# Two orders changed where a group of eight pairs begins in the last stage of a fused long convolution and rational feed-forward kernel

## What is computed

```python
    h_filt = h_mlp * window
    u = x * v
    ...
    y = np.fft.irfft(Uf * Hf[None, :, :], n=L, axis=1)[:, :S, :]
    return (x * y).astype(np.float32)
...
    h = x @ w_in                       # (24960, 128) @ (128, 2048)
    h2 = h * h
    h3 = h2 * h
    P = a[0] + a[1] * h + a[2] * h2 + a[3] * h3
    Q = 1.0 + np.abs(b[0]) * np.abs(h) + np.abs(b[1]) * h2
    g = P / (Q + 1e-06)
    return (g @ w_out).astype(np.float32)
```

## Time and profile before

| | |
|---|---|
| Median of three runs | 2089.32 us (2088.35 to 2089.32) |
| Profiled execution, its own time | 2086.96 us |
| Profiled execution, span from first to last instruction | 2084.5 us |
| Mean granted TensorE clock | 0.988 |
| PE busy | 1983.6 us (95%) |
| GpSimd busy | 1872.7 us (90%) |
| VectorE busy | 1826.2 us (88%) |
| ScalarE busy | 1825.9 us (88%) |

### The profile page before, as it was taken

One profiled execution on the slowest core, in us unless ns is written; L12 is line 12 of the kernel. 1 busy time (PEld: TensorE's weight loads), 2 busy tenths in 40 slices (PEclk: granted clock), 3 DMA queues, 4 the chain that ended last, 5 costly groups with the idle time before them and its releaser, 6 DMA issues. The chain is left out here.

```text
span 2084.5 us, 33029 instructions
## 1 busy us (share of the span) xinstructions
PE 1983.6 (95%) x8964; PEld 1466.1 (70%) x8964; DVE 1826.2 (88%) x2511; ACT 1825.9 (88%) x2671; POOL 1872.7 (90%) x1218
## 2 busy tenths in 40 slices
PE   7999799999969999999999999999999999999997
PEld 5777699999946666666666666666666666666664
DVE  5888688888859999999999989999899999999997
ACT  5888566666659999999999999999999999999998
POOL 4777588888839999999999999999999999999997
PEclk9999899999979999999999999999999999999999
DMA  7999876676540111111111111111111111111100
GB/s 202 307 309 310 229 176 174 176 182 169 140 108 21 44 33 32 32 32 33 32 32 32 37 33 33 33 32 48 35 43 32 32 33 32 32 32 32 33 13 13
DMA packets 66556, 176.34 MB, mean 85 GB/s; under 512 B 5191, under 2 KB 8975, under 8 KB 63519
## 3 DMA queue, kind: packets, MB, share of 16 engines
q1 hardware_dynamic: 66407, 174.67, 30.7%
HBM read 102.89 MB, written 71.76 MB: 84 GB/s over the span
## 5 line engine op out<-in xcount | busy, mean ns | idle before, releaser
L657 POOL TENSOR_TENSOR den<-slope,mag 128x832 f32<-128x832 f32 x480 | 947.0, 1973 | 0.0
L910 PE MATMUL acc_p<-g_s,w_out_k 128*128 128x416 f32 x1920 | 768.1, 522 | 48.8 <-DVE oT L830 22.9
L789 DVE SCALAR_TENSOR_TENSOR num<-square,level,h_p 128x832 f32<-128x832 f32 x480 | 517.6, 1078 | 82.3 <-ACT square L695 43.3
L649 POOL TENSOR_SCALAR slope<-mag,den_c 128x832 f32<-128x832 f32 x480 | 499.1, 1040 | 72.3 <-DVE mag L784 49.4
L910 PEld LDWEIGHTS acc_p<-g_s,w_out_k 128*128 128x128 f32 x1920 | 340.5, 189 | 296.0 <-issue 183.2
L822 DVE SCALAR_TENSOR_TENSOR g_s<-num,ratio,r_p 128x832 f32<-128x832 f32 x480 | 517.4, 1078 | 20.0 <-ACT r_p L711 4.6
L695 ACT ACTIVATE square<-h_p,centre 128x832 f32<-128x832 f32 x480 | 469.7, 979 | 41.7 <-DVE mag L784 24.2
L899 PE MATMUL h_p<-xy_hi,w_lo 128*128 128x416 f32 x960 | 460.5, 480 | 5.5 <-DVE num L789 2.8
L704 ACT ACTIVATE den<-den 128x832 f32<-128x832 f32 x480 | 442.4, 922 | 4.6 <-issue 2.9
L711 ACT ACTIVATE r_p<-den 128x832 f32<-128x832 f32 x480 | 428.2, 892 | 0.9 <-DVE g_s L822 0.7
L899 PE MATMUL h_p<-xy_lo,w_hi 128*128 128x416 f32 x960 | 338.5, 353 | 0.0
(11 more groups left out here) (79 smaller groups left out, 2792.8 us busy)
## 6 DMA issues: line engine op xcount, KB each, us to landing
bent<-bent_s SPq DMA_DIRECT2D x60, 576.0 KB, 5.8
bin_s<-bent SPq DMA_DIRECT2D x23, 1440.0 KB, 9.7
x_s<-in_x SPq DMA_DIRECT2D x59, 416.0 KB
vin_s<-back SPq DMA_DIRECT2D x29, 768.0 KB, 6.0
back<-back_s SPq DMA_DIRECT2D x23, 960.0 KB, 7.8
v_s<-in_v SPq DMA_DIRECT2D x30, 416.0 KB
out<-o_s SPq DMA_DIRECT2D x60, 208.0 KB
pos_s<-in_pos_emb SPq DMA_DIRECT2D x30, 88.0 KB
```

Of the source, the lines that this page charges most:

```text
L649: nc.gpsimd.tensor_scalar(slope[:, q % DEEP], mag[:, q % DEEP], den_c[:, 1:2], den_c[:, 0:1], ALU.mult, ALU.add).then_inc(slope_done, 1)
L657: nc.gpsimd.tensor_tensor(den[:, q % DEEP], slope[:, q % DEEP], mag[:, q % DEEP], ALU.mult).then_inc(den_done, 1)
L789: nc.vector.scalar_tensor_tensor(out=num[:, q % NUMS], in0=square[:, q % SQUARES], scalar=level[:], in1=h_p[:, q % 2, :, 0:TOK], op0=ALU.a ...
L910: mm = nc.tensor.matmul(acc_p[:, 0:TOK], w_out_k[:, ft], g_s[:, q % DEEP, t], start=(ft == 0), stop=(ft == FT - 1))
```

## The change

At an opening (m = 0 and m = 8) two orders are changed. VectorE does `times_x` (at m = 8) and `numerator` ahead of the copy of the sums. TensorE does `turn_in` (at m = 8) and `hidden` ahead of `project`. Nothing is added or removed, and each wait stays with its instruction.

```diff
@@ VectorE, step @@
                     activation(i, q)
+                    if more and m in TIMES_X:
+                        times_x(nxt + TIMES_X.index(m), i * (BLOCKS // SLOTS) + (q // BLOCK_PAIRS + 1) // SLOTS, s, TIMES_X.index(m))
+                    if ahead:
+                        numerator(i + (q + LEAD_E) // PER, (q + LEAD_E) % PER)
                     if m in SUMS:
                         c = blk * BATCH + SUMS.index(m) - 1
                         if positive(c + 1):
                             sums(c)
-                    if more and m in TIMES_X:
-                        times_x(nxt + TIMES_X.index(m), i * (BLOCKS // SLOTS) + (q // BLOCK_PAIRS + 1) // SLOTS, s, TIMES_X.index(m))
-                    if ahead:
-                        numerator(i + (q + LEAD_E) // PER, (q + LEAD_E) % PER)
@@ TensorE, step @@
-                    project(i, q)
+                    opens = m % PAIRS == 0
+                    if not opens:
+                        project(i, q)
                     nxt, s = (blk + 1) * 2, (q // BLOCK_PAIRS + 1) % SLOTS
                     if more and m in TURN_IN:
                         turn_in(nxt + TURN_IN.index(m))
                     if ahead:
                         hidden(i + (q + LEAD_H) // PER, (q + LEAD_H) % PER)
+                    if opens:
+                        project(i, q)
```

## The result

The changed kernel took 2092.63 us in the median of 13 runs (2090.57 to 2095.75), the kernel before 2088.49 us beside it (2086.29 to 2089.74). The ratio is 1.0024, with a 95% interval of 1.0016 to 1.0032. So the change made the kernel slower by a quarter of a per cent, where 0.42% faster was forecast.

The account below looks back on a forecast made before the run. A loop of ScalarE's chain and VectorE's steps through the magnitude was taken to set block time. A 13.7 us gain at m = 8 less 4.9 at m = 0 gave 8.8 us saved, 2080.5 us, range 2074 to 2088.5.

Parts of the forecast that it names:

- m = 8, VectorE: Openings at m = 8: the copy's wait for TensorE goes, a gain of 13.7 us over 29 openings.
- m = 0, VectorE: Openings at m = 0: the magnitude comes 0.13 us late in the loop, 0.23 outside, a loss of 4.9 us.
- m = 0, TensorE: Openings at m = 0: steps end 0.63 us later, about nothing lost; from above 0.2 us each, 5.8 us.
- The sum: Whole kernel: 13.7 - 4.9 = 8.8 us saved, 2080.5 us in the median, 0.42% less.
- The half clock at every m = 0: Rival: TensorE's clock drops at m = 0 openings, costing 41 us, about 2121 us; chance 0.05.
- nothing: Rival: the copy's wait comes back as another, of ScalarE or the numerator at m = 8; 2089.3 us; chance 0.08.
- GpSimd is the bound: Rival: both GpSimd pauses at m = 8 go, saving 29.6 us, 2059.7 us; chance 0.04.
- The transposes come too late for ScalarE at m = 2: Rival: at 0.2 us each the gain falls to 3.0 us, 2086.3; at 0.3 or more none; chance 0.2.
- The clock: TensorE's idle grows to about 1.26 us at m = 0, 3.2 at loop turns; one drop costs about 1.4 us.

Follow-up runs that it names:

- changed_less_products: The changed kernel with h of pairs 7 and 8 of each block summed from two products instead of three; 2080.39 us, ratio 0.9966 to the kernel before.
- m0_only: Both new orders, VectorE's and TensorE's, at m = 0 alone, with m = 8 as in the kernel before; 2108.34 us, ratio 1.0091.

## Why the prediction was wrong

**m = 8, VectorE: right.** The copy's wait cost 0.37 us in the block that I read, and the distance from `activation` to magnitude fell by that. The run with m = 8 alone gained 14.1 us (2088.72 - 2074.58), against a term of 13.7; in its trace it is 12.8 from the stage's first `activation` to its last.

**m = 0, VectorE: right.** The magnitude came 0.14 us later, against 0.13 in the loop. Over the 26 blocks between the first, the last and the two turns of the loop, the distances from one `activation` to the next give 4.9 us, as the term did for 29.

**m = 0, TensorE: this is the step that failed.** The text had it "about nothing, but close". Its own numbers were right: TensorE idle for 0.63 us more, the transposes 0.63 us later, ScalarE's copy to `o_s` not held up. The mistake was to follow the lateness to the next engine that waits, find a margin, and stop. I took it that TensorE would catch up, from the remark that it "runs up to two pairs ahead", for which I showed no row. It does not. Of the 0.63 us it still carries 0.43 in relation to VectorE at m = 4, and in its own distances it caught up 0.06 us in four pairs: 1310.55 - 1304.31 = 6.24 us for its first instruction of the opening, 6.18 at m = 3 and 4. It has the transposes of the output at m = 0 and the products of `rows` at m = 2 on top of its pairs. At m = 4 its result is wanted with next to no margin: in the kernel before, the transposes ended at 1318.14 + 0.52 = 1318.66 and the split started at 1318.75. The removed products confirm it, and m = 0 by itself repeats it. At 0.38 a block the term should have been 29 x 0.38 = 11 us of loss; over those 26 blocks the traces give 9.6 between m = 1 and m = 8.

The same step missed the stage's first opening. The prediction counted 29 openings at m = 0, those with a copy of the sums. The first of the 30 has no copy, but TensorE's order is new there too, and in the trace of the changed kernel that cost 3.4 us more.

**The sum.** With that term, 13.7 - 4.9 - 11 = 2.2 us of loss, and the two turns of the loop cost a little more, too:

```profile
1211.40:1214.80 3.40, 3.39 (x9) 2.58 (x10) 3.23 (x5) 3.10 (x5) 3.12 (x3) 0.56 0.00 0
1508.00:1511.40 3.40, 3.40 (x10) 2.24 (x9) 3.21 (x6) 3.00 (x5) 3.14 (x3) 0.61 0.00 0
```

These are windows of the kernel after, with the granted clock third from the end. It fell to its lower level after both turns, where before it fell after one. The two stretches of the earlier trace rows take 1237.85 - 1185.34 = 52.51 us and 1534.18 - 1481.74 = 52.44, against 52.11 and 50.75: 2.1 us more in all, of which 0.3 is that of two ordinary blocks. So about 4 us, and from the `activation` of pair 8 to the last one the two traces differ by 1438.95 - 1434.59 = 4.36. With the 3.4 us of the first opening the profiled pair differs by 7.8 in the stage. The medians differ by 4.1 only. Of the 13 executions of the changed kernel eight took 2090.57 to 2093.26 us and five, the profiled one among them, 2094.84 to 2095.75. It may be that the clock did not fall at the first opening in the eight, as it did not in changed_less_products; no trace of such an execution of the changed kernel shows it.

**The rivals.** The half clock at every m = 0 did not come, though it came at the stage's first, and "nothing" and "GpSimd is the bound" did not either. "The transposes come too late for ScalarE at m = 2" had the right thing, TensorE's delay, at the wrong place: it struck two steps later, at other transposes. Its range reached the measured loss only as an afterthought ("with 0.3 us or more nothing is left").

**The clock.** From 650 us on and outside the two turns, the granted clock of the kernel after reads 1.00, with the longer pause at all m = 0:

```profile
650.00:1205.00 555.00, 536.80 (x2097) 368.77 (x2096) 515.93 (x615) 540.99 (x775) 540.41 (x366) 1.00 0.13 34
1220.00:1500.00 280.00, 271.46 (x1061) 186.47 (x1059) 260.11 (x311) 272.52 (x391) 272.12 (x185) 1.00 0.14 35
1515.00:2060.00 545.00, 526.99 (x2058) 361.94 (x2057) 506.84 (x604) 531.58 (x762) 530.71 (x360) 1.00 0.13 32
```

So 27 pauses of 1.25 us cost no drop. In the Trainium skill, "TensorE: Matmul & The Clock Gate", section "HAM oscillation — how this bites in real kernels", the pauses that bring the half clock back are waits for a DMA of some 3 to 5 us. The pauses here are shorter, so this trace neither bears the section out nor speaks against it.

## What to carry to other kernels

When a step makes an engine late, ask where it catches up before asking who waits next: follow the lateness down that engine's own order until a pause swallows it, and look at every result that is handed over on the way. A margin of 0.1 us at a handover four steps on decides as much as the one next to the edit. Look as well at the first place where the edit applies: a stage that is only starting can pay another price there than in its steady course. And where one edit is made at two places, price and run the two apart: here one gained 14 us and the other lost 20.

## What the runs showed of the hardware

Where the hardware loop turns back, TensorE was idle for 2.6 and 2.7 us before, and for 3.37 and 3.25 us in the changed kernel, and its clock fell to the lower level after one turn of the two before and after both in the changed kernel. Over all nine traces the loop turns back 18 times. A drop followed each of the seven pauses of more than 3 us (3.05 to 3.37), and eight of the eleven shorter ones (2.48 to 2.74). So no length of pause parts the two here.

A drop can also come elsewhere. At the stage's first opening it came in the changed kernel and in m0_only, with a pause of 2.30 us, and not in changed_less_products, with one of 1.70. It never came at the 27 pauses of 1.25 us.
